# Strassen's seven block products in the first MoE layer, token operands in DRAM

## The reference

```python
# attention: batch 4, heads 8, sequence 576, head size 64, mask by blocks of 64
scores = where(block_i >= block_j, q @ k.T / 8, -1e9)
attn_out = softmax(scores) @ v
x = attn_out.transpose(0, 2, 1, 3).reshape(2304, 512)
# first layer: 4 experts, w1[e] is 512 x 1024, w2[e] is 1024 x 512
p = domain_probs / (domain_probs.sum(-1, keepdims=True) + 1e-9)
for e in range(4):
    out += p[:, e:e+1] * (maximum(x @ w1[e], 0) @ w2[e])
# second layer, on that output
h = out @ w_in                               # 512 x 1024
solu = h * softmax(h)
return (layernorm(solu, no bias) * g_ln) @ w_out
```

## Time and profile before

| what | value |
|---|---|
| median of 3 runs | 1252.47 us (1251.94 to 1254.22) |
| the profiled execution's own time | 1254.11 us |
| its span in the trace | 1252.3 us |
| TensorE matmul busy | 1230.2 us, 98% |
| VectorE, ScalarE, GpSimd busy | 500.0, 348.9, 144.3 us |
| moved by DMA | 53.86 MB |

### The profile page before, as it was taken

The page is one execution under the profiler, slowest core; times in us unless marked ns, Lnnn a source line. Parts: engine busy times, 40 slices in busy tenths (PEclk is TensorE's granted clock), DMA queues, the critical chain, the costliest instruction groups (busy, mean ns, idle before and its releaser), DMA issues.

```text
span 1252.3 us, 18036 instructions
## 1 busy us (share of the span) xinstructions
PE 1230.2 (98%) x6536; PEld 1103.1 (88%) x6536; DVE 500.0 (40%) x917; ACT 348.9 (28%) x808; POOL 144.3 (12%) x149
## 2 busy tenths in 40 slices
PE   7999999999999999999999999999999999999997
PEld 6999998899999999999999999999999977888886
DVE  6878886321213321222412111422121356655552
ACT  6777776211112211111311111311111232322221
POOL 4667652000000000000000000000000000010100
PEclk9999999999999999999999999999999999999999
DMA  6667662300002200000400000310000100000000
GB/s 165 152 161 163 147 132 73 102 1 0 0 0 59 76 0 0 0 0 8 126 0 0 0 0 0 92 43 0 0 0 0 42 26 18 17 25 17 25 18 33
DMA packets 76009, 53.86 MB, mean 43 GB/s; under 512 B 38864, under 2 KB 60368, under 8 KB 75984
## 3 DMA queue, kind: packets, MB, share of 16 engines
q1 hardware_dynamic: 75984, 53.54, 16.6%
HBM read 39.89 MB, written 4.79 MB: 36 GB/s over the span
## 4 chain that ended last, share of the span: by engine, by line
PE 95%; issue 2%; DVE 1%; ACT 1%; DMA 0%; POOL 0%; POOLq 0%; ACTq 0%; DVEq 0%
PE s L960 65%; PE outp L960 24%; PE ring L971 4%; PE ring L1162 1%; PE outp L1124 1%; ACT pr L544 0%; ACT ptr_h L549 0%; DMA k_raw<-in_k 0%; DVE ptr_l L715 0%; DVE h_max L904 0%; DVE ln L934 0%; PE ring L973 0%; DVE k_l L720 0%; DVE sums_e L726 0%; DVE solu L921 0%
## 5 line engine op out<-in xcount | busy, mean ns | idle before, releaser
L857 DVE SCALAR_TENSOR_TENSOR hid_l<-s,hid_h 128x384 fp32r<-128x384 f32 x192 | 107.0, 557 | 521.3 <-ACT hid_h L635 521.3
L635 ACT ACTIVATE hid_h<-s 128x384 fp32r<-128x384 f32 x192 | 94.2, 491 | 655.5 <-PE s L960 655.5
L960 PE MATMUL s<-x_l,w_h 128*128 (+1 forms) x768 | 258.5, 337 | 0.0
L960 PE MATMUL s<-x_h,w_h 128*128 (+1 forms) x768 | 258.2, 336 | 0.0
L960 PE MATMUL s<-x_h,w_l 128*128 (+1 forms) x768 | 258.1, 336 | 0.0
L960 PE MATMUL s<-w_h,hid_h 128*128 128x512 f32 x384 | 153.3, 399 | 0.0
L960 PE MATMUL s<-w_l,hid_h 128*128 128x512 f32 x384 | 151.0, 393 | 0.0
L960 PEld LDWEIGHTS s<-x_h,w_h 128*128 128x128 f32 x768 | 144.3, 188 | 6.5
L960 PEld LDWEIGHTS s<-x_h,w_l 128*128 128x128 f32 x768 | 144.4, 188 | 6.2
L960 PE MATMUL s<-w_h,hid_l 128*128 128x512 f32 x384 | 149.1, 388 | 0.0
L960 PEld LDWEIGHTS s<-x_l,w_h 128*128 128x128 f32 x768 | 144.4, 188 | 0.0
(11 more groups left out here) (111 smaller groups left out, 1832.3 us busy)
## 6 DMA issues: line engine op xcount, KB each, us to landing
stage<-in_moe_w SPq DMA_DIRECT2D x64, 256.0 KB, 2.9
qb<-q_hl SPq DMA_DIRECT2D x30, 288.0 KB, 5.3
k_raw<-in_k SPq DMA_DIRECT2D x16, 288.0 KB, 3.1
q_over<-in_q SPq DMA_DIRECT2D x16, 288.0 KB, 3.4
r_sb<-r_scratch SPq DMA_DIRECT2D x32, 144.0 KB, 3.2
out<-o_sb SPq DMA_DIRECT2D x18, 256.0 KB, 2.0
v_nat<-in_v SPq DMA_DIRECT2D x16, 256.0 KB, 2.6
stage<-in_moe_w_in SPq DMA_DIRECT2D x8, 256.0 KB, 3.1
```

The source lines that it names most:

```text
L635: act.activation(hid_h[f % 2][:, :], s01[:, 512 * (f % 2):512 * (f % 2) + GROUP], ACT.Relu).then_inc(hid_high, 1)
L857: dve.scalar_tensor_tensor(out=hid_l[f % 2][:, :], in0=s01[:, 512 * (f % 2):512 * (f % 2) + GROUP], scalar=0.0, in1=hid_h[f % 2][:, :].bit ...
L960: last = pe.matmul(target, x, y, start=start and i == 0, stop=stop and i == 2)
```

## The change

Two groups of 384 tokens, two halves of the depth (512 = 2 x 256) and two hidden chunks (f and f+4) form a 2x2 by 2x2 block product. `up` computes it by Strassen's method (in the form with shared sums) by seven block products instead of eight; A is w1 transposed, B the tokens. One **unit** m is an expert, a "super" of 768 tokens (3 of them) and a pair of chunks (4 of them): 48 units. The sums of w1 blocks and of token blocks are formed before, on GpSimd, and split into high and low like all operands; the results c11, c12, c21 and c22 are put together by VectorE from PSUM and SBUF. `down` is unchanged in its arithmetic: four parts a unit, one for each block of the result. For half of the parts other banks are used, so all eight banks are in use.

The seven token operands of a super take `xr`, 7 x 1536 values of 4 bytes in each partition. They are loaded again from DRAM (`x_stash`) for every super after the first, one DMA of 786 KB for each operand. Attention outputs go to DRAM (`x_dram`, one DMA of 295 KB a pair) instead of `x_h` and `x_l`; the pairs now come in batch order, so that the first super's tokens are complete after eight pairs. All loops of the first layer, and ScalarE's over the pairs, are written out instead of looped. The second layer computes the same, with w2's chunks in another order.

```diff
+    PRODUCTS = {"m1": (A11, B11), "m6": (S2, T2), "m2": (A12, B21), "m7": (S3, T3), "m5": (S1, T1),
+                "m4": (A22, T4), "m3": (S4, B22)}
...
@@ sync
-                return p % BATCH * HEADS + 2 * (p // BATCH)
+                return 2 * p
...
+            def store_x(p):
+                sp.wait_ge(right_scaled, 2 * (p + 1))
+                sp.wait_ge(left_scaled, p + 1)
...
+                sp.dma_start(x_dram[c * P:(c + 1) * P, b * SEQ:(b + 1) * SEQ], x_n[:, :]).then_inc(x_stored, 16)
...
+            def load_operands(n):
+                sg = n % SUPERS
...
+                for name in ORDER:
+                    s = PRODUCTS[name][1]
+                    if 0 < n < SUPERS:
+                        sp.wait_ge(tmp_stored[round_of[s] % 2], 16 * (tmp_uses(sg, 1, round_of[s]) + 1))
+                    sp.wait_ge(prod_done, made(HALF_F * n - 1, name))
+                    sp.dma_start(xr[:, s * SLOT:(s + 1) * SLOT].bitcast(f32), x_stash[sg, :, s * SLOT:(s + 1) * SLOT]
+                                 ).then_inc(ring_loaded[s], 16)
...
                 spread_r(p)
+                if p >= 1:
+                    store_x(p - 1)
                 if p + 4 < PAIRS:
                     load_q(p + 4)
+                if p in (1, 3, 5, 7):
...
+                    load1(w1[0, :, :], v_)
+                if p == 9:
+                    load_x(0, 0)
+                if p == 11:
+                    load_x(0, 1)
...
+            sp.wait_ge(x_low, 2 * NR)
+            sp.dma_start(x_stash[0, :, :], xr[:, :].bitcast(f32)).then_inc(stash_stored, 16)
+            store_x(PAIRS - 1)
+            for sg in (1, 2):
+                load_x(sg, 0)
...
+                stash_round(sg, 0, 0)
...
+                load_operands(sg)
@@ gpsimd
+            def w1_add(e, v):
...
+                pool.tensor_tensor(s1, a21, a22, ALU.add).then_inc(w1_sums, 1)
+                pool.tensor_tensor(s3_, a11, a21, ALU.subtract).then_inc(w1_sums, 1)
...
+            def w1_low_sums(e, v):
...
+                pool.tensor_tensor(operand1(w1s_l[u], S1, 4), sums1[:, :], operand1(w1s_h[u], S1, 4).bitcast(f32),
...
+                if p in (10, 12):
+                    x_add(0, p // 2 - 5)
+                    x_low_part(0, p // 2 - 5, 0)
+                    x_low_part(0, p // 2 - 5, 1)
@@ scalar
+            def early(p):
+                if p in (2, 4, 6, 8):
+                    w1_cast_plain(0, p // 2 - 1, 0)
+                if p in (10, 11, 12, 13):
+                    x_cast(0, p // 2 - 5, p % 2 * 2)
...
-                if not first:
-                    output_high(p - 1)
+                early(p)
...
+                split2(0, 0)
+                split2(0, 1)
                 high(T67, p, par)
+                copy_m1(0)
...
+            def copy_m1(m):
+                act.wait_ge(prod_done, made(m, "m1"))
+                if m >= 1:
+                    act.wait_ge(hid_done, hid_no(m - 1, "c21"))
+                act.activation(m1[:, :], bank_x(m), ACT.Copy).then_inc(m1_copied, 1)
...
+                if m >= 1:
+                    copy_m1(m)
+                    after_m1(e, sg, u)
+                hid_c11(m)
+                if m >= 1:
+                    after_c11(e, sg, u)
+                hid_rest(m, "c22", 2, u3)
...
+                hid_rest(m, "c21", 1, m1)
+                hid_rest(m, "c12", 3, u2)
@@ vector
                 if not (isinstance(p, int) and p == 0):
-                    dve.wait_ge(x_done, p)
+                    dve.wait_ge(x_stored, 16 * p)
...
+                if n >= 1 and u == 1:
+                    accumulate(n - 1, 1, downs(m - 2, 4))
+                if m >= 1:
+                    make_u2(m)
+                hid_low(m, "c11", 0, bank_x(m))
...
+                make_u3(m)
...
+                    accumulate(n - 1, 0, downs(m - 1, 2))
+                dve.wait_ge(prod_done, made(m, "m5"))
+                dve.wait_ge(comb_done, combined(m, "u3"))
+                dve.tensor_tensor(u3[:, :], bank_x(m), u3[:, :], ALU.add).then_inc(comb_done, 1)
+                dve.wait_ge(prod_done, made(m, "m4"))
+                dve.tensor_tensor(m1[:, :], bank_y(m), m1[:, :], ALU.add).then_inc(comb_done, 1)
+                hid_low(m, "c22", 2, u3[:, :])
+                hid_low(m, "c21", 1, m1[:, :])
+                dve.wait_ge(prod_done, made(m, "m3"))
+                dve.tensor_tensor(u2[:, :], bank_x(m), u2[:, :], ALU.add).then_inc(comb_done, 1)
+                hid_low(m, "c12", 3, u2[:, :])
@@ tensor
+                for t in range(2):
+                    a = tuple(w[u][:, k * BLK + t * P:k * BLK + (t + 1) * P] for w in (w1s_h, w1s_l))
+                    last = sharing(target, a, (operand_x(s, t, 0), operand_x(s, t, 1)),
+                                   name in ("m1", "m6", "m5") and t == 0, name in ("m2", "m4", "m3") and t == 1)
...
+            def unit(m):
+                up(m, "m1")
+                down(m - 1, 1)
+                up(m, "m6")
+                up(m, "m2")
+                down(m - 1, 2)
+                up(m, "m7")
+                down(m - 1, 3)
+                up(m, "m5")
+                up(m, "m4")
+                down(m - 1, 4)
+                up(m, "m3")
```

More of the change, by code:

```diff
@@ L652, in _ @@
[L652 to L663 removed]
+                source = s01[:, 0:512] if isinstance(t, int) and t == 0 else outp[:, 512:1024]
@@ L1096, in down_part, with sharing @@
-            def down_part(e, g, f, first=False):
-                done = (e * GROUPS + g) * FC
-                pe.wait_ge(w2_ready, e * FC + f + 1)
-                pe.wait_ge(hid_done, done + f + 1)
+            def sharing(target, a, b, start, stop):
+                passes = ((a[0], b[0]), (a[1], b[0]), (a[0], b[1]))
+                for i, (x, y) in enumerate(passes):
+                    last = pe.matmul(target, x, y, start=start and i == 0, stop=stop and i == 2, skip_group_check=True)
+                return last
@@ new lines, in down @@
+            def down(m, part):
+                n, u = m // HALF_F, m % HALF_F
+                e = n // SUPERS
+                slot = part - 1
+                j = 2 * u + (part in (2, 3))
+                pe.wait_ge(w2_ready, FC * e + j + 1)
+                pe.wait_ge(hid_done, hid_no(m, {1: "c11", 2: "c21", 3: "c22", 4: "c12"}[part]))
+                if u == 0 and part == 1:
+                    if n >= 1:
+                        pe.wait_ge(acc_done, 2 * GT * (n - 1) + GT)
+                    else:
+                        pe.wait_ge(left_scaled, PAIRS)
+                if u == 0 and part == 3:
+                    if n >= 1:
+                        pe.wait_ge(acc_done, 2 * GT * n)
+                    else:
+                        pe.wait_ge(right_scaled, 2 * PAIRS)
@@ L1101, in down_part @@
                 for t in range(GT):
-                    if first and t == GT - 1:
-                        pe.wait_ge(right_scaled, 2 * PAIRS)
-                    last = product(down[t][:, 0:D], tuple(x[f % 2][:, t * P:(t + 1) * P] for x in (hid_h, hid_l)),
-                                   (chunk2(w2_h, f), chunk2(w2_l, f)), f == 0, f == FC - 1)
+                    last = product((down_a if part < 3 else down_b)[t],
+                                   tuple(x[:, t * P:(t + 1) * P] for x in hid[slot]),
+                                   (chunk2(w2_h, j), chunk2(w2_l, j)),
+                                   u == 0 and part in (1, 3), u == HALF_F - 1 and part in (2, 4))
@@ L1119, in turn_y @@
             def turn_y(t):
                 pe.wait_ge(y_copied, t + 1)
-                if not (isinstance(t, int) and t == 0):
+                first = isinstance(t, int) and t == 0
+                if first:
+                    pe.wait_ge(comb_done, combined(UNITS - 1, "c21"))
+                else:
                     pe.wait_ge(y_done, t)
+                if isinstance(t, int) and t == 1:
+                    pe.wait_ge(acc_done, EXPERTS * TT - 2 * GT + 1)
+                bank = s01[:, 0:512] if first else outp[:, 512:1024]
@@ L1132, in _ @@
-            pe.wait_ge(x_done, PAIRS)
-            with pe.Fori(1, GROUPS) as g:
-                group(0, g)
-            with pe.Fori(1, EXPERTS - 1) as e:
-                with pe.Fori(0, GROUPS) as g:
-                    group(e, g)
-            with pe.Fori(0, GROUPS - 1) as g:
-                group(EXPERTS - 1, g)
-            group(EXPERTS - 1, GROUPS - 1, last=True)
+            for m in range(1, UNITS):
+                unit(m)
+            down(UNITS - 1, 1)
+            turn_y(0)
+            for part in (2, 3, 4):
+                down(UNITS - 1, part)
```

713 lines of the change are left out of this document (503 added, 210 removed).

## The result

The kernel with the change took **1204.66 us** (median of 4 runs, 1204.52 to 1206.34), the kernel before 1253.06 (median of 4, 1251.94 to 1254.22): a ratio of 0.9617, 95% interval 0.960 to 0.9633. The forecast was 1203.8. The profiled execution took 1204.52 us, of which the span is 1202.6.

A forecast was written before the change was run, and what follows sets the result against it. TensorE's matmuls were taken to bound the kernel: -50.2 us for those removed, +1.0 for GpSimd beside VectorE and +0.5 at the seams make -48.7, so 1203.8 us against 1252.47; forecast range 1200 to 1210, chance 0.67.

The forecast's parts named there:

- The matmuls removed: First layer's `up`: 288 fewer matmuls of 384 columns at 0.1742 us each, 50.2 us less; a unit takes 15.6 us.
- The new waits: TensorE's waits in a unit for operands VectorE and ScalarE combine: 0 taken, bounds 0 and 0.3 us a unit, 14 us.
- over 2 us late: In a unit, TensorE waits for work queued behind a waiting VectorE add only when that work is this late.
- GpSimd beside VectorE: First layer: GpSimd's sums and splits block VectorE operations with two SBUF inputs; +1.0 us in all, bounds 0 and 16 us.
- The reload: Loading seven token operands again before every super but the first: 0 taken; first expert's late operands bounded 0 and 10 us.
- T of 2.3: Predicted us for one 786 KB operand load in the reload, at 339 GB/s; up to 3.9 us was held harmless.
- stall = 7T - 27.1: TensorE's predicted wait in us per reload, 11 times, with T the time per operand load; from T = 4.5 the gain is gone.
- rival C: Reload through one queue too slow, so the kernel becomes slower than before: 1336 us at 141 GB/s; chance 0.04.
- Landing within 4 us of issue: Predicted sign in the first layer: each load of `xr` from `x_stash` lands within 4 us of its issue.
- Attention: Attention steps stay at 12.67 us despite the new stores and moved work: 0 taken, bounds -2 and +6 us.
- The seams: Last attention step: casts and a copy before ScalarE's high parts, +0.5 us; second layer's start and end 0, bounds -0.5 and +2.
- Code: TensorE's 47 units as straight code instead of a loop: 0 taken for instruction fetch, +10 us if 30 further loads cost 0.32 each.

## Why the prediction was right

**The matmuls removed: -50.2.** Right. 288 fewer, 15.60 us a unit as worked out; putting 288 back costs 1.04 us a unit, 50.4 in all by the medians.

**The new waits: 0.** Right, and for the reason given: VectorE has 2.15 us of slack ahead of m4, where "over 2 us late" stood, and by the trace as much at its other combinations from unit 3 on.

**GpSimd beside VectorE: +1.0.** The right size, 0 to 0.6 us, at another place. The prediction looked at u = 0 of experts 1 to 3, with splits and accumulations; no unit there is longer. It left out that the shares' small divisions read SBUF twice, too, and that units 1 and 2 are the tight ones. A blocked operation's length is set by GpSimd's operation and not by its own: three of the four divisions of 18 values, 0.18 us each alone, took 0.75, 0.94 and 1.77 us, and each ended within 0.04 us of the end of a GpSimd operation. That the total came so near is in part luck, since it hangs on one meeting of these operations in unit 1 that four other runs did not have.

**The reload: 0.** Right, with a smaller margin than worked out. In the first expert, where the seven loads follow one another in the queue, an operand lands every 1.9 us. In the nine later reloads it is one every 2.7, because each load waits for its slot; SP issues the seven over 14.9 us, as the products of the unit before end. First expert, then a later reload, and a window of the first:

```profile
262.10 9.45 SPq L549 DMA_DIRECT2D xr<-x_stash  x7
...
381.44 14.88 SPq L549 DMA_DIRECT2D xr<-x_stash  x7
```

```profile
270.00:281.00 11.00, 11.00 (x57) 9.92 (x56) 3.71 (x7) 1.43 (x3) 0.00 (x0) 1.00 1.00 409
```

The last operand is there 7.7 to 8.8 us ahead of its m3 in the nine, and 4.6 and 6.0 us ahead in the first expert, where the operands are made late; the prediction's T of 2.3 would give 11. So the first expert is the tight place. The rule stall = 7T - 27.1 has the right slope and the right sign of danger, and is 0.5 to 2.3 us too low on both sides of its edge. The clock's fall, which the prediction left out of rival C, comes in such waits but adds little there, as the next landing mostly decides. "Landing within 4 us of issue" was wrong: 4.1 to 4.3 us for the first load of a later reload, 6.0 in the median, because a load queues behind the one before. For the end of a row of loads T and the time of the last issue count, not this.

**Attention: 0.** The profiled executions differ by 1.5 us, but not by the change. The first step (from the first turned probabilities of one pair to those of the next) took 13.90 us before and 12.26 after, and the windows show why, first before, then after:

```profile
16.00:18.00 2.00, 1.73 (x8) 1.43 (x8) 1.85 (x5) 1.14 (x4) 0.27 (x1) 0.73 0.90 289
18.00:20.00 2.00, 2.00 (x10) 1.81 (x9) 1.10 (x2) 0.24 (x1) 1.92 (x2) 0.50 1.06 188
```

```profile
18.00:20.00 2.00, 2.00 (x18) 2.00 (x16) 1.20 (x3) 1.85 (x5) 1.92 (x2) 1.00 1.08 186
```

TensorE had waited 2.07 us for a query load before, 1.40 after. Of the runs here, all with the new order of pairs, the three with waits of 2.54 to 2.60 us at this place had the low clock and a step of 13.6. The six with waits of 1.40 to 1.93 had neither, with steps of 12.3. The two with 1.96 and 2.00 kept the clock, but their step took 13.76, with a further wait of 0.87 for VectorE. So it is chance, mostly of a load, and it is most of what the profiled execution before stood above its median. By the medians the change is worth 1253.06 - 1204.66 = 48.4 us, and the sum said 48.7. The sizes agree better than either number is known, since one fall of the clock is 1.6 us. The steps after the first are 12.65 to 12.85 us, but for one of 13.01 and the last; the store lands 2.2 us or more ahead of VectorE.

**The seams: +0.5.** One new gap of 0.4 us on issue in the last attention step. The three gaps at the second layer's start are the same as before (1.48, 0.68 and 1.5 us).

**Code: 0.** Right. The instruction queue has 37 loads where 14 were the earlier trace rows, and no gap in 46 units answers to one. The Trainium skill (Runtime: NRT & Kernel Launch, "Instruction fetch mechanics") has straight code fetched ahead; the trace agrees.

## What to carry to other kernels

Where TensorE's chain is solid, price a change by the distance between starts, and prove each new wait harmless by its slack; the slack is in the trace as the distance from a result's end to its reader's start, and repeated operations showed it to 0.2 us. Ask of every wait that may appear whether it is long enough to take the clock with it: here one of 1.1 us cost its length, one of 3.5 us 1.5 us more. But where the next operand is late anyway, the lower clock costs little. Place VectorE's operations with two SBUF inputs, tiny ones above all, where GpSimd is idle or where nobody waits.

## What was not expected of the hardware

- The clock after one wait. In the twelve traces no single wait of TensorE up to 2.00 us, once it had reached 2.4 GHz, was followed by a fall; one of 1.92 us was that came shortly after another of 1.46. (The last 2 us of each run are left out here.) After waits of 2.07 to 2.60 us it fell to 1.2 GHz in 12 of 19 cases, after 2.86 to 3.31 in 11 of 16, after all 24 of 3.37 us and more. It stayed there for 3.4 us, sometimes 6.8, and where nothing else was late 1.5 or 2.8 us were lost. One and the same wait, 3.21 us in every run, was followed by a fall in eight traces of twelve.
- Four VectorE operations of 18 values took 3.75 us beside GpSimd's (0.84 alone), one of 384 up to 1.82 (0.55).
- One queue moved 415 GB/s in loads and copies with rows of 6 KB, for 24 us at a stretch, and TensorE's matmuls beside it kept 174 ns between starts.
